# Eight weight-block sums of the first MLP's second layer moved from VectorE to GpSimd

## What is computed

```python
def _attn_ref(q, k, v, g_norm):
    kv = np.einsum('bhsd,bhse->bhde', k, v)
    out = np.einsum('bhsd,bhde->bhse', q, kv)
    rms = np.sqrt(np.mean(out * out, axis=-1, keepdims=True) + 1e-06)
    return out / rms * g_norm

def _moe_ref(x, w_ch1, w_ch2):          # first MLP
    mixed = np.real(np.fft.fft(np.fft.fft(x, axis=1), axis=2))
    u = x + mixed
    un = (u - mean(u)) / np.sqrt(var(u) + 1e-06)
    return u + np.maximum(un @ w_ch1, 0.0) @ w_ch2

def _moe2_ref(x, U, V, w_ch1, w_ch2):   # second MLP
    u = x + ((x.transpose(0, 2, 1) @ U) @ V).transpose(0, 2, 1)
    return u + np.maximum(u @ w_ch1, 0.0) @ w_ch2
```

## Time and profile before

| | us |
|---|---|
| median of 3 runs (lowest, highest) | 1747.55 (1746.29, 1749.99) |
| the profiled execution, its own time | 1749.69 |
| its span, first to last instruction | 1747.9 |
| PE busy | 1695.9 (97%) |
| DVE busy | 1377.2 (79%) |
| ACT busy | 802.0 (46%) |
| POOL busy | 223.1 (13%) |

### The profile page before, as it was taken

The page is one execution under the profiler, slowest core; times in us unless marked ns, Lnnn a source line. Parts: engine busy times, 40 slices in busy tenths (PEclk is TensorE's granted clock), DMA queues, the critical chain, the costliest instruction groups (busy, mean ns, idle before and its releaser), DMA issues.

```text
span 1747.9 us, 27408 instructions
## 1 busy us (share of the span) xinstructions
PE 1695.9 (97%) x10712; PEld 1643.6 (94%) x10712; DVE 1377.2 (79%) x1741; ACT 802.0 (46%) x1163; POOL 223.1 (13%) x170
## 2 busy tenths in 40 slices
PE   5999989899999999999999999999999999999999
PEld 5888779899999999999999999999999999999999
DVE  5999989988887987986976867957857758659567
ACT  2344646545445445445444445434434444343343
POOL 0464320020020020020110110100100100100200
PEclk9999999999999999999999999999999999999999
DMA  8785569998988898898986777966867767767663
GB/s 252 253 278 193 212 240 363 382 343 303 328 312 307 325 318 303 321 323 306 317 284 241 287 235 267 335 226 243 281 220 251 267 237 253 265 223 252 226 249 122
DMA packets 118753, 478.15 MB, mean 274 GB/s; under 512 B 12897, under 2 KB 40865, under 8 KB 77922
## 3 DMA queue, kind: packets, MB, share of 16 engines
q1 hardware_dynamic: 118258, 475.22, 77.1%
q10 hardware_dynamic: 368, 1.18, 0.2%
HBM read 396.14 MB, written 78.64 MB: 272 GB/s over the span
## 4 chain that ended last, share of the span: by engine, by line
PE 77%; DVE 16%; issue 4%; DMA 3%; ACT 1%; SPq 0%; DVEq 0%; ACTq 0%
PE pair L977 11%; PE pair L978 11%; PE pair L979 11%; PE pair L1008 6%; PE pair L1009 6%; PE pair L1010 6%; PE pair L997 5%; PE pair L1000 5%; PE pair L999 5%; DVE t_lo L1628 4%; DMA sseq_sb<-s_seq 2%; PE pair L750 2%; DVE t_raw L1647 2%; PE pair L771 2%; PE tr_ps L865 1%
## 5 line engine op out<-in xcount | busy, mean ns | idle before, releaser
L977 PE MATMUL pair<-t_hi,w_sb 128*128 128x384 f32 x1344 | 461.6, 343 | 9.1 <-DVE h_sb L1665 7.2
L978 PE MATMUL pair<-t_lo,w_sb 128*128 128x384 f32 x1344 | 456.1, 339 | 0.0
L979 PE MATMUL pair<-t_hi,w_sb 128*128 128x384 f32 x1344 | 455.8, 339 | 0.0
L1295 ACT ACTIVATE t_hi<-t_raw 128x768 fp32r<-128x768 f32 x240 | 203.1, 847 | 280.0 <-DVE t_raw L1647 279.9
L1628 DVE TENSOR_TENSOR t_lo<-t_raw,t_hi 128x768 fp32r<-128x768 f32 x300 | 303.1, 1016 | 16.0 <-ACT t_hi L1283 14.6
L1874 POOL TENSOR_TENSOR t_raw<-a_sb 128x768 f32<-128x768 f32 x60 | 135.7, 2265 | 1277.5 <-PE pair L1000 553.6
L997 PE MATMUL pair<-w_sb,t_hi 128*128 128x256 f32 x1008 | 285.5, 283 | 8.7 <-DVE t_lo L1628 7.8
L999 PE MATMUL pair<-w_sb,t_hi 128*128 128x256 f32 x1008 | 282.7, 280 | 0.0
L1000 PE MATMUL pair<-w_sb,t_lo 128*128 128x256 f32 x1008 | 282.6, 280 | 0.0
L977 PEld LDWEIGHTS pair<-t_hi,w_sb 128*128 128x128 f32 x1344 | 253.3, 188 | 17.3 <-issue 12.7
L978 PEld LDWEIGHTS pair<-t_lo,w_sb 128*128 128x128 f32 x1344 | 253.2, 188 | 2.6
(11 more groups left out here) (189 smaller groups left out, 2196.3 us busy)
## 6 DMA issues: line engine op xcount, KB each, us to landing
w_sb<-wc SPq DMA_DIRECT2D x263, 1024.0 KB, 5.6
wc<-w_sb SPq DMA_DIRECT2D x25, 1024.0 KB, 6.6
w_raw<-wr1a SPq DMA_DIRECT2D x24, 512.0 KB, 7.6
w_raw<-wr1b SPq DMA_DIRECT2D x24, 512.0 KB, 4.1
w_raw<-wr2a SPq DMA_DIRECT2D x10, 1024.0 KB, 8.1
wc<-pb_v SPq DMA_DIRECT2D x16, 640.0 KB, 6.8
q_sb<-q_t SPq DMA_DIRECT2D x8, 1152.0 KB, 9.1
u_dram<-x_sb SPq DMA_DIRECT2D x24, 384.0 KB, 4.7
```

The source lines that it names most:

```text
L977: nc.tensor.matmul(ps, w_hi, hi[:, x, :], start=(fresh and x == 0), stop=False, skip_group_check=True)
L978: nc.tensor.matmul(ps, w_hi, lo[:, x, :], start=False, stop=False, skip_group_check=True)
L979: last = nc.tensor.matmul(ps, w_lo, hi[:, x, :], start=False, stop=(x == 1), skip_group_check=True)
L1295: nc.scalar.activation(t_hi[r][:, :, :], t_raw[r][:, :, :], ACT.Copy).then_inc(hi_ready, 1)
```

## The change

Eight of the eleven dn-layer sums of group 0, those of slots 16, 17, 18, 19 (products 5 and 1) and 24, 25, 26, 27 (products 7 and 6), are made by POOL and no longer by DVE. `len(UP_SLOTS) + 2` is 16. POOL waits, before each, for all earlier sums (`w_summed`), because two engines now count on one semaphore. Nothing else is changed; the code from L1863 on moves down by two lines.

```diff
@@ in @block.vector
                         if n > 1 and NSTEP * g + t == split_step(n):
                             split_slot_lo(n)
-                        if 1 < n < NSLOT and NSTEP * g + t == max(0, split_step(n) - 2) and summed_slot(n):
+                        if 1 < n < len(UP_SLOTS) + 2 and NSTEP * g + t == max(0, split_step(n) - 2) and summed_slot(n):
                             sum_slot(n)
@@ in @block.gpsimd, sum_slot
                 pool.wait_ge(w_loaded[r], 16 * (n // RING + 1))
+                if n < NSLOT:
+                    pool.wait_ge(w_summed, len([m for m in RAW_SLOTS if m < n and summed_slot(m)]))
                 x, y, op = slot_sum(w_raw[r], slot_product(n)[0])
@@ in @block.gpsimd, the loop over groups and steps
                     for n in RAW_SLOTS:
-                        if n > NSLOT and NSTEP * g + t == split_step(n) - 2 and summed_slot(n):
+                        if n >= len(UP_SLOTS) + 2 and NSTEP * g + t == split_step(n) - 2 and summed_slot(n):
                             sum_slot(n)
```

## The result

The changed kernel takes 1754.91 us (median of 20 runs, 1750.13 to 1760.03), the kernel before in the same comparison 1747.26 (20 runs, 1743.34 to 1752.44). The ratio is 1.0041, 95% interval 1.0032 to 1.0050: slower by 0.41%, about 7 us. The profiled execution took 1758.1 us, its span is 1756.3. The forecast was 1752.0 in 1747.5 to 1757.0: the side is right, the size was 4.5 of some 7 us. 1754.91 lies above the 1750 to 1754 that the prediction gave its own case (held as costed); it is inside the range because that was drawn wide enough for the starved case, which did not occur.

The account below looks back on a forecast made before the run. DVE was taken as the bound, PE waiting 8.2 us from 319.8 to 366.0. Net costs +0.2 (slots 16-19), +0.8 (slot 24) and +3.5 (25-27) gave +4.5 on 1747.55: 1752.0 us, range 1747.5 to 1757.0.

Parts of the forecast that it names:

- held as costed: The forecast's own case: POOL sums hold DVE as costed, +4.5 us in all, 1750 to 1754; chance 0.48.
- the starved case: Rival: full DVE keeps POOL out, slots 25 to 27 wait until DVE idles; about +8, 1755.5; chance 0.2.
- DVE as the bound from 319.8 us on, one for one: 319.8 to 366.0 us: DVE busy throughout, PE loses 8.2 us; changes to DVE's chain reach PE about one for one.
- 2.3 us a sum: Each POOL sum stops DVE for 2.3 us, less DVE time meanwhile on one-SBUF-input operations.
- Slot 24 partly covered by the read at 326.19: Slot 24, landed at 322.5: PSUM read near, 1.9 us held taken, net +0.8.
- the late four were costed at +4.3: Late slots: slot 24 net +0.8; slots 25, 26, 27 fully held, +3.5.
- Early four, +0.2: Slots 16 to 19, about 290.5 to 303 us: 4.8 held, 4.6 removed, net +0.2.
- The +5.5: Total if the scaling at 298.01, contending as two-port `tensor_scalar`, would not cover slot 19's sum: about +5.5 us.
- The signs it named: Eight POOL sums, 290-350 us; DVE operations 1.7-3.2 us; DVE full; group 0's end 4-5 later; `t_lo` waits 12-13.
- The rivals within 0.2% and faster: Nothing measurable: holds mostly covered, about +2, 1749.5, chance 0.21. Faster: holds rare, DVE relieved, 1740.5, chance 0.11.

Follow-up runs that it names:

- late four: Only the sums of slots 24 to 27 on GpSimd, 16 to 19 left on VectorE, against the kernel before: ratio 1.0020, dn half 76.0 us.
- early four: Only the sums of slots 16 to 19 on GpSimd, 24 to 27 on VectorE, against the kernel before: ratio 1.0017, dn half 74.6 us.
- the memsets: Kernel before plus four unneeded write-only GpSimd memsets of 128x2048 beside the late slots: 1748.51 us in a single run, dn half 71.9.
- four other runs: Added unneeded sums 1758.88 us, added copies 1752.01, both on the kernel before; changed kernel with slot 19's sum delayed, 1.0040; slots 24-27 on GpSimd, VectorE-released, 1.0027.
- the one run of the late four with it: Sums of slots 24 to 27 alone on GpSimd, each also released by a VectorE `t_lo`, against the kernel before: ratio 1.0027, dn half 76.4 us.
- the run with slot 19's sum after the scaling: The changed kernel, with slot 19's sum also waiting for the next group's token scaling; against the kernel before: ratio 1.0040, dn half 78.2 us.
- that run: Kernel before with sums of slots 16 to 19 made by accumulating DMAs issued from GpSimd: 1746.49 us, ratio 0.9989, dn half 71.5 us.

## Why the prediction was right on the side and short in size

- **DVE as the bound from 319.8 us on, one for one**: right for the late four. Net of holds 8.6 - 4.6 = 4.0 us, dn half +4.1.
- **2.3 us a sum**: measured 2.0 to 2.2 where fully held. Right.
- **Slot 24 partly covered by the read at 326.19**: it was not. The sum asked in the middle of the `t_raw` before and got in at the split: 2.2 us, not 1.9. Slot 25's got the read's cover in its stead and still held the next `t_lo` 2.04, since it asked only 0.2 us before the read ended. Together the late four were costed at +4.3 and cost +4.1.
- **Early four, +0.2**: the term that failed. It had two faults. The small one: it counted the scaling as cover, though a `tensor_scalar` between SBUF tiles is held like a two-input operation, 1.9 us where 1.2 was costed; the other three holds came out as costed (0.9, 1.3 and 1.3 for 0.8, 1.4 and 1.4). That makes 5.5 us held instead of 4.8, +0.9 net. The large one: it let only `t_lo` carry DVE's delay to PE. The sentence "whatever the change adds to DVE's chain or takes from it there arrives at PE about one for one" overlooked that the scaling has a reader of its own, PE's transpose, which stands in PE's queue in front of the dn steps with less than 1 us of lead: before, the scalings were over at 299.0 and the transpose began at 299.90. It waited 3.0 us, and the dn step behind it took 3.9 us in place of 2.3 at the lower clock, while the `t_lo` of that step lay ready since 297.35. Of these 4.6 us 1.5 reached VectorE as idle time. PE made good most of the rest: it ran without a wait for `t_lo` up to 329 us, where it had begun to wait at 320 before. The early four cost 2.7 us in all. Costed 0.2, measured 2.7: this is the whole miss.
- **The rule of the Trainium skill ("SBUF — State Buffer", Who interferes with whom)** on `tensor_scalar` in its two-port mode was right to count it as contending: 0.17 us became 1.07, and 1.00 became 2.91. It had been set aside for want of a row. The +5.5 worked out by it is near the net of the holds, +5.0, and misses the transpose as well. The same section of the Trainium skill has it that an operation of GpSimd which only writes does not collide with two-input reads; the memsets bear that out. The rule of the Trainium skill there that the first to issue has the ports is not what the runs show: one that asked was passed by VectorE for up to 32 us.
- **The signs it named**: the eight rows on POOL and the lengthened operations on DVE are there. PE's waits for `t_lo` are 10.0 us, not 12 to 13; the 3.0 us of the transpose bring the total to 13.0 at a place that was not foreseen. DVE is not full to the end but idle for 1.5 us, and the end of group 0 comes 7.1 us later, not 4 to 5.
- **The starved rival (0.2)**: it did not happen in the change; every sum began within 1 us of asking. The mechanism is real, as four other runs show, but its price was put too high: in the one run of the late four with it, after one idle of 3.4 us the rest was as in the held case, +4.5 in place of the +7.3 that the prediction gave three such sums.
- **The rivals within 0.2% and faster**: they needed holds that are covered or short. Two of the eight had the cover of a product read (1.34 us held) and one was shorter than the sum removed (0.90 us); the late four had neither.

## What to carry to other kernels

GpSimd is no spare VectorE while VectorE runs operations with two SBUF inputs: a sum that costs VectorE 1.14 us cost it 2.0 to 2.2 us when GpSimd made it beside such operations. Cost such a move as an exclusive hold, and then ask for every VectorE operation that is pushed later who reads it: a reader without a lead adds a loss of its own, here a transpose, some 2 of the 7 us. Memsets, and the part of a sum that fell beside reads of PSUM, cost VectorE nothing here.

## What the runs showed of the hardware that was not expected

- GpSimd can be shut out of SBUF reads for as long as VectorE runs two-SBUF-input operations back to back: 32 us for a sum of 2.4 us, and the same for a one-input copy of 1.04 us. A single VectorE operation with an input from PSUM, or a short idle, lets it in.
- A `tensor_scalar` on two elements per partition, 0.17 us long, took 1.07 us beside a GpSimd sum.
- A wait of 3.0 us on TensorE ended at 303.1 us, and from 304 to 308 us the granted clock was 0.61; a wait of 1.1 us at the same place, in the run with slot 19's sum after the scaling, left it at 1.00 there.
- An accumulating DMA of 512 KB issued from GpSimd landed 9.8 us after its issue (median of four) beside DMA engines that were busy throughout (1.03 by the view of windows, 290.4 to 319.8 us of that run).
